# Product for u in a fused mLSTM, gMLP and mixture-of-experts kernel: the low part of x's last 64 rows as pairs of 64-row products

## The reference, cut to what matters

```
h = relu(x @ w_in)                    # w_in is 320 x 1024
u, v = h[..., :512], h[..., 512:]
v_n = (v - mean) / sqrt(var + 1e-6)
v_s = w_spatial @ v_n + b_spatial
gated = u * v_s
x = gated @ w_out
```

## Time and profile before

| | us |
|---|---|
| median of 3 runs | 372.16 (370.95, 372.16, 375.73) |
| the profiled execution | 373.6 |
| its span, first to last instruction | 371.6 |
| PE busy | 356.7 (96%) |
| DVE busy | 282.3 (76%) |
| ACT busy | 207.3 (56%) |
| POOL busy | 190.1 (51%) |
| L1609, PE, 192 matmuls | 24.5 |

### The profile page before, as it was taken

How to read it: one execution, slowest core, us unless ns; L and a number is a source line. 1 busy time by engine, 2 the same in 40 slices (tenths; PEclk the granted TensorE clock), 3 DMA queues, 4 the chain that set the end, 5 groups by cost and what they waited for, 6 DMA issues and landing times.

```text
span 371.6 us, 7371 instructions
## 1 busy us (share of the span) xinstructions
PE 356.7 (96%) x2413; PEld 307.7 (83%) x2413; DVE 282.3 (76%) x536; ACT 207.3 (56%) x455; POOL 190.1 (51%) x212
## 2 busy tenths in 40 slices
PE   6989999999999999999999999999999999999992
PEld 3977999899999898999999854577888888888882
DVE  3699876887878799536175676898889888889882
ACT  2875564564555492115211352777788778777880
POOL 3578535281714303123121346777777777777752
PEclk9999999999999999999999999999999999999998
DMA  8988559392944047001498385697522222121110
GB/s 119 235 167 208 108 160 181 86 203 69 208 94 145 2 137 260 0 23 42 141 373 337 120 275 152 196 315 288 154 76 74 80 68 65 57 68 33 43 38 17
DMA packets 71495, 50.32 MB, mean 135 GB/s; under 512 B 52682, under 2 KB 63211, under 8 KB 71452
## 3 DMA queue, kind: packets, MB, share of 16 engines
q1 hardware_dynamic: 67574, 39.44, 40.1%
q0 software_dynamic: 1808, 5.31, 4.7%
q10 hardware_dynamic: 2070, 5.03, 4.0%
HBM read 45.40 MB, written 4.87 MB: 135 GB/s over the span
## 4 chain that ended last, share of the span: by engine, by line
PE 81%; DVE 7%; ACT 3%; DMA 3%; issue 2%; SPq 1%; POOL 1%; DVEq 0%; POOLq 0%; ACTq 0%
PE psum L1729 13%; PE psum L1929 13%; PE psum L1894 10%; PE psum L1609 5%; PE psum L1809 5%; PE psum L1598 5%; PE psum L1906 4%; PE psum L1562 4%; PE psum L1914 4%; PE psum L1552 3%; PE psum L1574 2%; PE psum L1581 2%; PE psum L1639 2%; DMA early<-m_rows 1%; PE psum L1875 1%
## 5 line engine op out<-in xcount | busy, mean ns | idle before, releaser
L720 POOL TENSOR_TENSOR late<-w1m,late 128x512 fp32r<-128x512 f32 x47 | 61.3, 1319 | 20.8 <-ACT late L990 20.7
L1443 DVE TENSOR_TENSOR late<-arena,late 128x640 fp32r<-128x640 f32 x60 | 59.0, 1002 | 8.6 <-ACT late L1001 6.8
L1729 PE MATMUL psum<-halves 128*128 128x384 f32 x288 | 54.5, 340 | 0.0
L990 ACT ACTIVATE late<-w1m 128x512 fp32r x62 | 38.9, 632 | 24.4 <-PE psum L1894 16.1
L1929 PE MATMUL psum<-late,xt_high_low 128*128 128x320 f32 x280 | 50.9, 313 | 0.0
L1894 PE MATMUL psum<-late 128*128 128x512 f32 x180 | 49.1, 405 | 1.0 <-POOL late L720 0.8
L1729 PEld LDWEIGHTS psum<-halves 128*128 128x128 f32 x288 | 49.3, 188 | 0.1
L1001 ACT ACTIVATE late<-arena 128x640 fp32r x60 | 44.0, 738 | 6.3 <-PE psum L1929 3.1
L1929 PEld LDWEIGHTS psum<-late,xt_high_low 128*128 128x128 f32 x280 | 42.8, 188 | 0.0
L1894 PEld LDWEIGHTS psum<-late 128*128 128x128 f32 x180 | 31.7, 188 | 8.6 <-POOL late L720 2.5
L583 POOL TENSOR_SCALAR early<-early 128x320 f32<-128x320 f32 x12 | 12.1, 1011 | 34.9 <-ACT early L807 34.9
(11 more groups left out here) (278 smaller groups left out, 730.4 us busy)
## 6 DMA issues: line engine op xcount, KB each, us to landing
arena<-in_moe_w_dram SPq DMA_DIRECT2D x8, 1280.0 KB, 8.4
w1m<-in_moe_w_dram SPq DMA_DIRECT2D x8, 1024.0 KB, 9.0
early<-m_rows SPq DMA_DIRECT2D x10, 512.0 KB, 4.8
w_rest<-in_moe_w_dram SPq DMA_DIRECT2D x38, 128.0 KB, 2.6
arena<-in_moe_w_spatial_dram ACTq DMA_DIRECT2D x6, 384.0 KB, 3.8
x_rows<-early SPq DMA_DIRECT2D x12, 192.0 KB, 2.1
heads<-in_q_dram SPq DMA_DIRECT2D x12, 160.0 KB, 4.7
heads<-in_k_dram SPq DMA_DIRECT2D x12, 160.0 KB, 4.5
```

The lines of the kernel that those rows point to most:

```text
L720: g.tensor_tensor(w1l[k % 2], w1m[:, ds(e * 2 * FF + k % 2 * FF + k // 2 * 512, 512)], w1h[k % 2].bitcast(fp32), ALU.subtract).then_inc(m_ ...
L990: A.activation(w1h[k % 2], w1m[:, ds(e * 2 * FF + k % 2 * FF + k // 2 * 512, 512)], ACT.Copy).then_inc(m_1h, 1)
L1443: V.tensor_tensor(w2l[:, i * QW:(i + 1) * QW], w2s[:, ds(e * NFT * DM + i * QW, QW)], w2h[:, i * QW:(i + 1) * QW].bitcast(fp32), ALU.subtr ...
L1729: last = T.matmul(PS[n % 4][:, 0:HALF], v_[s_][:, dt * P:(dt + 1) * P], w_[half][:, s_ * HALF:(s_ + 1) * HALF], start=s_ == 0 and i == 0, ...
```

## The change

The first seven products of each output stay. The eighth, low x of the third block by `wih`, had 128 rows: x_low x (w_high + w_low). It becomes a product of 64 rows, x_low x w_high. For two outputs, `dt` = 0 and 2, then 1 and 3, the two 64-row products stand behind each other: one in partitions 0 to 63 into bank 7, one in partitions 64 to 127 into the other bank. For the second half a copy of w_high is needed in partitions 64 to 127, for outputs 2 and 3 only: ACT makes it once (`wih_third`, 64 x 256). The outputs' order becomes 0, 2, 1, 3; `u_ps` rises by 2 at the end, where before it rose by 1 in the middle and by 1 at the end; and the wait for `tmp_ok[0]` now stands behind the seventh matmul, where it stood behind the sixteenth. There are 32 matmul instructions to a call before and after.

```diff
+        wih_third = halves[:, BEHIND + GW:BEHIND + GW + FH // 2]
...
+        third_hi = sem("third_hi")
...
                     w_in_high(2)
+                    A.activation(wih_third[REM:P, :], wi[REM:P, KD - 1, FH // 2:FH], ACT.Copy).then_inc(third_hi, 1)
                     act.wait_ge(g_t, G_STATE)
...
             def project_both(c):
 
                 past(pe, tmp_ok[1], c)
-                for dt in range(NDT):
-                    if dt == NDT // 2 and c < NC - 1:
-                        pe.wait_ge(tmp_ok[0], c + 1)
-                    to = PS[(7, u_bank(c))[dt // 2]][:, dt % 2 * 2 * P:(dt % 2 + 1) * 2 * P]
-                    for i, (x_, w_, m) in enumerate(TERMS):
-                        last = T.matmul(to, w_[:, m, dt * P:(dt + 1) * P], x_[:, m, :, :],
-                                        start=i == 0, stop=i == len(TERMS) - 1)
-                    if dt % 2:
-                        last.then_inc(u_ps, 1)
+                if c == 0:
+                    pe.wait_ge(third_hi, 1)
+                to = [PS[bank][:, n * 2 * P:(n + 1) * 2 * P] for bank in (7, u_bank(c)) for n in range(2)]
+                for pair in range(NDT // 2):
+                    for dt in (pair, pair + NDT // 2):
+                        if dt == NDT // 2 and c < NC - 1:
+                            pe.wait_ge(tmp_ok[0], c + 1)
+                        for i, (x_, w_, m) in enumerate(TERMS[:-1]):
+                            T.matmul(to[dt], w_[:, m, dt * P:(dt + 1) * P], x_[:, m, :, :], start=i == 0, stop=False)
+                    T.matmul(to[pair], wih[0:REM, KD - 1, pair * P:(pair + 1) * P], xtl[0:REM, KD - 1, :, :],
+                             start=False, stop=True)
+                    last = T.matmul(to[pair + NDT // 2], wih_third[REM:P, pair * P:(pair + 1) * P],
+                                    xtl[REM:P, KD - 1, :, :], start=False, stop=True)
+                last.then_inc(u_ps, 2)
```

More of the change, by code:

```diff
@@ L229, in mlstm_gmlp_moe_kernel @@
         behind = halves[:, BEHIND:BEHIND + GW]
+        wih_third = halves[:, BEHIND + GW:BEHIND + GW + FH // 2]
         gth, gtl = [[t.rearrange("p (k s) -> p k s", k=NDT) for t in two] for two in (
             [xt_high_low[:, i * GW:(i + 1) * GW] for i in range(2)], [xt_high_low[:, 2 * GW:3 * GW], behind])]
-        assert (NC - FRONT_LOW) * FH <= KD * F1 and BEHIND + GW <= E * 2 * FF and 3 * GW <= 2 * XT2
+        assert (NC - FRONT_LOW) * FH <= KD * F1 and BEHIND + GW + FH // 2 <= E * 2 * FF and 3 * GW <= 2 * XT2
         W1_HALF = range((FRONT + 2 * FF - 1) // (2 * FF), (FRONT + WI_AT + KD * F1) // (2 * FF))
```

## The result

Over 22 runs of each, the changed kernel has a median of 374.34 us (373.81 to 379.05) and the kernel before 373.05 us (370.84 to 376.34). The ratio is 1.0055, with a 95% interval from 1.0035 to 1.0075: slower by about 2.1 us. (The ratio is worked out over the undisturbed runs and is not the quotient of the two medians, which differ by 1.3 us.)

The account below looks back on a forecast made before the run. PE was taken as the bound. Per pair 0.20 + 0.18 + 0.11 - 0.24 = +0.25 us, times ten counting pairs = +2.5 us on the median 372.2: 374.7 us, slower by 0.7%; range for all 372.5 to 377.0.

Parts of the forecast that it names:

- What bounds: From 36 to 137 us PE is busy 100.11 of 101 us, so a matmul slot or hole costs its whole length.
- The slots removed, and the pair put there: In each call of the product for u, per two outputs: two slots go, 0.24 us; one 64-row pair comes, 0.11 us.
- The joints: PE's changes between 128-row and 64-row matmuls around each pair: 0.20 us lost on the way in, 0.18 out.
- The low bound from `fold`: Round trip between 128-row and 64-row matmuls read from fold: 0.30 us, making +0.17 us per pair of outputs.
- before, each call had one joint: Before the change each call had only the joint out of the scores, and it stays; every new pair pays both ways.
- What is swallowed: Second call's +0.5 us vanishes in PE's 0.55 us wait for ACT at L1574, so ten of twelve pairs count.
- The edits at nothing: Late u_ps release, earlier tmp_ok[0] wait, ACT's copy (about 0.3 us) and early third_hi: all covered, no cost.
- No joint: Rival, 10%: fp32r pairs pay no joint in the calls, each gains 0.13 us; -1.3 us, 370.9 us.
- one after the other: Rival, 8%: the pair's two 64-row products do not run together, 0.36 us a pair; +3.8 us, 376.0 us.
- the late release bites: Rival, 6%: ACT's L827, L830, L813 behind the call delay PE, up to 0.5 us in five calls; 377.2 us.
- absorbed: Rival, 6%: some later wait for a transfer takes up the delay; 372.2 us.
- the sum: Product for u: +0.25 us per pair of outputs, ten pairs counting, +2.5 us; 376.1 us from the profiled execution's 373.6.

Follow-up runs that it names:

- the grouped kernel: Kernel before with fold's four 64-row parts placed two by two next to each other; ratio 1.0005, stretch from spatial on 226.44 us for 227.03.
- late_release: Kernel before with one edit: u_ps rises by 2 at the call's end, not 1 in the middle and 1 at the end; ratio 0.9971.
- copy_only: Kernel before with only ACT's 64 x 256 copy and PE's wait for it added; ratio 0.9984.
- the kernel with one half of the array: Changed kernel with both 64-row products of a pair in partitions 0 to 63; ratio 1.0091 to the kernel before.
- the two controls: Kernel before with only u_ps's release by 2 at the end, 0.9971; changed kernel with the eighth products again over 128 rows, 0.9967.
- the second profile of the old kernel: Kernel before, unchanged, timed against itself; ratio 0.9987, span of the profiled execution 369.6 us.
- a kernel that saves nothing: Changed kernel with all other edits kept but the eighth product of each output again over 128 rows; ratio 0.9967 to the kernel before.
- around_and_fold: Kernel before with 64-row pairs on both sides of the scores in five calls and fold's 64-row parts grouped two by two; ratio 0.9971, median 370.93 us.
- around_scores: Against the kernel before: in the first five calls one 64-row pair ahead of the scores and one behind, last call all 128-row; ratio 0.9982.

## Why the prediction was right

The forecast was +2.5 us on 372.2 us, the median of the first three runs: 374.7 us. Measured are 374.34 us and a ratio of +0.55% (2.1 us); the sums in the table give +2.1 to +2.4 us. The mechanism and the size per call were right. That the absolute time came within 0.4 us is in part luck: over 22 runs the kernel before has a median of 373.05 us, 0.9 us above the base that was used, and the growth came out smaller than 2.5 us (2.1 by the ratio, 1.3 between the medians), so the two errors cancel in part.

- **What bounds.** PE was the bound, and a hole in PE costs its length: the columns of the table move by what the calls move, outside the second call.
- **The slots removed, and the pair put there.** 0.24 us for two slots was exact (L1617 x2, 0.24). The pair of 256 columns, for which I had only a pair of 128 fp32 columns, takes 0.12 us and not 0.11, and both run at once.
- **The joints.** 0.20 in and 0.18 out, taken from fp32 scores, hold for fp32r: from the last full matmul (39.09) to the first full one behind the pair, recorded at 39.62 and streaming 0.10 us later, it is 0.63 us where three steps of 0.12 stood, so 0.27 a pair; over a whole call the chain says 0.48, or 0.24 a pair, for 0.25. The low bound from `fold`, 0.30 for a round trip, was too low here, but right for `fold` itself, as the grouped kernel shows. That the weight load starts "only when that matmul has left the array" is a reading: the records show it 0.21 us behind the start of the last full matmul and 0.07 ahead of that matmul's modelled end. And "before, each call had one joint" holds for five calls; the sixth stands behind 128-row transposes and had none, which changes nothing in the sum.
- **What is swallowed.** That the second call's loss vanishes in the wait for ACT was right: 8.83 or 9.09 us there became 8.33, and taking that call's loss away brought the wait back. The size is loose. The idle gap of 0.55 us understates the room, since the column is 0.82 us over the usual 8.27 in the same execution; and the wait varies, from 0.33 us (`late_release`) to 0.92 (`copy_only`). Against the longer wait of the first execution the kernel lost 2.1 us in all, against the second 2.4.
- **The edits at nothing.** Release and copy, alone, and all the edits together cost nothing that the traces show; the earlier wait was tried only with the others. L813 was late by the half us that I worked out, and covered.
- **The rivals.** "No joint" and "one after the other" fell to the trace and to the kernel with one half of the array; "the late release bites" to the two controls; "absorbed" holds for one call of six and no more.
- **What I did not see:** that the profiled execution of before had a slow start. The profile after, 372.3 us in span, looks like +0.7 us beside it, and would have seemed a refutation of the sum; the second profile of the old kernel makes it +2.8, of which 2.4 from the second transposes of x on.

The rule of "TensorE: Matmul & The Clock Gate" in the Trainium skill, "Part 3: Packing small matmuls", that matmuls in different row groups run at once, is borne out: recorded starts 39.30 and 39.31. What it gains here is 0.12 us a pair. "TensorEngine Tiling (Array Packing)" in the Trainium skill, "Key Properties", says that a change of tiling mode drains TensorE; the trace agrees, and prices the change at about 0.2 us each way.

## What to carry to other kernels

A pair of 64-row products saves one slot (0.12 us here for 256 columns), and the two changes between 128-row and 64-row matmuls cost 0.38. So it pays only next to work that has 64 rows anyway, or where several pairs stand together: two still lost 0.12 to 0.15 us a call, and by these prices it takes four to gain (an estimate, not tried). Look for such joints in the chain as a first matmul that is recorded 0.10 us too long and a weight load that doesn't start under the matmul before, and group them, as `fold` did for 0.6 us. A saving upstream of a wait can be lost in it, and a loss hidden by it: both happened behind the second call. For changes of 0.1 to 1% read stage lengths from the traces, of more than one execution: most repeated to 0.01 us, where five rounds of whole runs gave 0.9967 for a kernel that saves nothing.

## What the runs showed of the hardware

- Near the start of the program, between 7.7 and 12.2 us, the granted clock is at its half level (1.2 GHz) for some 3.4 us in some executions and not in others of the same kernel: mean 0.87 or 1.00 over the first 13 us. The first transposes of x start at 21.5 to 21.9 us with it and at 19.7 to 20.4 without, as much as the change itself; of the 1.8 us between the two executions of the kernel before, about 0.6 were there before the clock fell. Why it falls was not tried.
- The recorded clock does not tell all of it. `around_and_fold` reads 1.00 over those 13 us, yet eight of its matmuls (L1544, from 8.90 us) take 1.91 us where `around_scores` has 1.16 (from 8.41 us), and its first transposes of x start latest of all, at 22.78 us.
- One execution (a single pair behind the scores) had such a stretch from 66.8 to 70.2 us. PE had stood idle for 0.79 us until 65.8 us, in the wait for ACT, and was busy throughout from there to the fall; other executions had a wait of 0.7 to 0.8 us there and kept the full clock.
- Matmuls of 64 rows in fp32r and in fp32 follow each other without a hole: the scores behind a pair take 0.89 us for eight pairs of 0.11, and the pair behind the scores adds 0.11. So the change of rows, not of type, is what costs.
